# Delta rule in 32- and 48-row products on TensorE, with 16x16 inverses joined by products

## The reference

```python
k_n = k / (norm(k) + 1e-06)                  # batch 4, 8 heads, 768 tokens, head 48
for t in range(S):                           # the delta rule, state 48x48 per head
    y[t] = q[t] @ state
    v_old = state.T @ k_n[t]
    state = state + beta[t] * outer(k_n[t], v[t] - v_old)
x = y as (3072 tokens, 384)
h = x @ w_in;  x = (P(h) / (Q(h) + 1e-6)) @ w_out     # 384 -> 2048 -> 384, rational unit
h = x @ w_in2; out = (h * tanh(softplus(h))) @ w_out2 # same sizes
```

## Time and profile before

| | us |
|---|---|
| median of 3 runs | 1171.37 (1165.88 to 1178.27) |
| the profiled execution, its time | 1173.33 |
| its span | 1171.5 |
| TensorE, busy | 1071.8 (91%) |
| VectorE, busy | 950.9 (81%) |
| ScalarE, busy | 766.7 (65%) |
| GpSimd, busy | 171.6 (15%) |
| granted TensorE clock, mean | 0.943 of full speed |

### The profile page before, as it was taken

One profiled execution on the slowest core, in us unless ns is written; L12 is line 12 of the kernel. 1 busy time (PEld: TensorE's weight loads), 2 busy tenths in 40 slices (PEclk: granted clock), 3 DMA queues, 4 the chain that ended last, 5 costly groups with the idle time before them and its releaser, 6 DMA issues.

```text
span 1171.5 us, 22278 instructions
## 1 busy us (share of the span) xinstructions
PE 1071.8 (91%) x9321; PEld 870.6 (74%) x9366; DVE 950.9 (81%) x1045; ACT 766.7 (65%) x1039; POOL 171.6 (15%) x328
## 2 busy tenths in 40 slices
PE   5388999999888899999999999889999999999997
PEld 3276877877766677787787777668888888888885
DVE  4965567554569999999999999999887888878785
ACT  1535456466367687777867768687676767667664
POOL 2088787780000000000000000000000000000000
PEclk7588889996899999999999999999999999999999
DMA  7625447343021010000101003230010101010000
GB/s 198 185 62 159 137 111 192 97 110 124 22 87 54 1 55 1 25 30 0 54 0 54 1 1 108 81 107 28 1 55 1 54 0 54 1 54 1 25 4 27
DMA packets 30489, 69.03 MB, mean 59 GB/s; under 512 B 4160, under 2 KB 11840, under 8 KB 30400
## 3 DMA queue, kind: packets, MB, share of 16 engines
q1 hardware_dynamic: 30144, 66.98, 19.2%
q10 hardware_dynamic: 256, 0.79, 0.3%
HBM read 53.60 MB, written 14.16 MB: 58 GB/s over the span
## 4 chain that ended last, share of the span: by engine, by line
DVE 35%; PE 33%; issue 3%; ACT 2%; DVEq 0%; ACTq 0%
PE o_ps L837 6%; PE o_ps L838 5%; PE o_ps L839 5%; PE h_ps L837 5%; PE h_ps L839 5%; PE h_ps L838 5%; DVE val L1022 5%; DVE val L1041 5%; DVE val L1054 5%; DVE g_lo L1060 5%; DVE den L1014 5%; DVE den L1049 5%; DVE pa L1020 4%; PE h_ps L881 0%; ACT den L901 0%
## 5 line engine op out<-in xcount | busy, mean ns | idle before, releaser
L910 ACT ACTIVATE g_hi<-val 128x1024 fp32r<-128x1024 f32 x96 | 102.0, 1062 | 99.7 <-DVE val L1054 93.6
L837 PE MATMUL o_ps<-g_hi,w_hi_late 128*128 128x512 f32 x288 | 116.8, 405 | 20.5 <-DVE g_lo L1060 20.4
L837 PE MATMUL o_ps<-g_hi,w_hi_early 128*128 128x512 f32 x288 | 114.8, 399 | 14.3 <-ACT stage L947 9.2
L1054 DVE SCALAR_TENSOR_TENSOR val<-den,val 128x1024 f32<-128x1024 f32 x96 | 117.7, 1226 | 10.7 <-DVE den L1049 0.5
L1060 DVE SCALAR_TENSOR_TENSOR g_lo<-val,g_hi 128x1024 fp32r<-128x1024 f32 x96 | 117.6, 1225 | 1.6 <-ACT g_hi L910 1.5
L837 PE MATMUL h_ps<-x_hi,w_hi_early 128*128 128x512 f32 x288 | 112.2, 390 | 2.0 <-DVE val L1022 2.0
L837 PE MATMUL h_ps<-x_hi,w_hi_late 128*128 128x512 f32 x288 | 112.5, 391 | 1.6 <-DVE w_lo_late L88 1.6
L838 PE MATMUL o_ps<-g_lo,w_hi_late 128*128 128x512 f32 x288 | 113.8, 395 | 0.0
L839 PE MATMUL o_ps<-g_hi,w_lo_early 128*128 128x512 f32 x288 | 113.5, 394 | 0.0
L838 PE MATMUL o_ps<-g_lo,w_hi_early 128*128 128x512 f32 x288 | 113.4, 394 | 0.0
L839 PE MATMUL o_ps<-g_hi,w_lo_late 128*128 128x512 f32 x288 | 113.3, 393 | 0.0
(11 more groups left out here) (111 smaller groups left out, 2360.2 us busy)
## 6 DMA issues: line engine op xcount, KB each, us to landing
w_raw<-w SPq DMA_DIRECT2D x16, 768.0 KB, 6.1
kv_run<-kv_n SPq DMA_DIRECT2D x24, 384.0 KB, 4.6
x_raw<-x_dram SPq DMA_DIRECT2D x12, 768.0 KB, 5.8
kq_run<-kq_t SPq DMA_DIRECT2D x44, 192.0 KB, 3.5
kq_gram<-kq_t SPq DMA_DIRECT2D x40, 192.0 KB, 6.7
x_dram<-stage SPq DMA_DIRECT2D x24, 192.0 KB, 4.0
x_dram<-stage SPq DMA_DIRECT2D x6, 768.0 KB, 4.3
out<-stage SPq DMA_DIRECT2D x5, 768.0 KB, 4.1
```

The source lines that it names most:

```text
L837: nc.tensor.matmul(dst, hi, rhs_hi, start=first, stop=False)
L910: act_fn(g_hi[:, n % 2], val[:, n % 2], ACT.Copy, scale=-1.0).then_inc(g_hi_ready, 1)
L1054: dve_stt(val[:, e], den[:, e], 2.0, val[:, e], ALU.subtract, ALU.mult).then_inc(g_ready, 1)
```

## The change

The block-diagonal operands are gone. `solve`, `within` and the two halves of `update` work on the 32 rows of one batch at a time, 16 products each for 4 heads x 4 batches; `q_state` takes q as the loaded operand, so y comes out by token, in the upper half of the same two banks (`ky_ps`) that `k_state` writes. `turn_y` turns the y of the step before by two products with an identity matrix; ScalarE copies y before and after it. `update` is cut in halves with `turn_y` between them. Only the two diagonal 16x16 blocks are inverted by `substitute` (30 operations); the block between them is made by two rounds of products on TensorE (`join`, k = 0 and 1 for one half of the heads, 2 and 3 for the other) with a masked copy on ScalarE and a sum on VectorE. One buffer `kq` with three slots replaces `kq_gram` and `kq_run`, so k and q are loaded once. The warm products of the steps and the second burst are gone. `scale_gram` of tau 1 moves ahead of the first step. y is stored with one DMA for each half tau in place of two. In the diff, runs of removed lines are left out (the functions that held them are printed above), as are the first eight columns of indentation.

```diff
--- before.py
+++ after.py
...
+HC = C // 2
+BLK = HC * C + HC
 BANK = 512
+Y_AT = BANK // 2
...
-WARM = 2
...
+STEPS = 2 * (HC - 1)
+HALF = CG // 2
+def substitute(eng, tt, own, step, done):
+    n, x = blocks(n_turned), blocks(inv)
+    for r in range(HC - 1, 0, -1):
+        shape = [P, 2, r, HC - r]
+        prod = inv_t[:, own, :, 0:r, r:HC]
         if done:
             eng.wait_ge(step, done)
...
+        tt(prod, n[:, :, r, 0:r].unsqueeze(3).broadcast_to(shape),
+           x[:, :, r, r:HC].unsqueeze(2).broadcast_to(shape), ALU.mult).then_inc(step, 1)
         eng.wait_ge(step, done + 1)
-        tt(inv[:, j % 2, 0:r, r:C], inv[:, j % 2, 0:r, r:C], prod, ALU.subtract).then_inc(step, 1)
+        tt(x[:, :, 0:r, r:HC], x[:, :, 0:r, r:HC], prod, ALU.subtract).then_inc(step, 1)
...
+    load_kv(0, 0)
+    sp.wait_ge(ident_zeroed, 1)
+    for b in range(B):
+        sp.dma_start(ident[quad(b), quad(b)],
+                     consts[0:1, C + B:C + B + C * C].rearrange("o (i k) -> (o i) k", k=C)).then_inc(ident_loaded, 16)
+    load_norm(2)
...
+    def join(j, k):
+        h = k // 2
+        if k == 0:
+            pe.wait_ge(z_diag_ready, j + 1)
+            if j and j + 1 < T:
+                pe.wait_ge(gram_used, 4 * (j + 1) + 4)
+            elif j:
+                pe.wait_ge(joined, 2 * j)
+        elif k == 1:
+            pe.wait_ge(x_ready, TURNS * j + TURNS)
+            pe.wait_ge(r_ready, 2 * j + 1)
+        elif k == 2:
+            pe.wait_ge(joined, 2 * j + 1)
+        else:
+            pe.wait_ge(r_ready, 2 * j + 2)
+        by_event()
+        for n in range(HALF):
+            m = HALF * h + n
+            for b in range(B):
+                left, right = ((n_mat[quad(b), j % 2, m], z_diag[quad(b), m]) if k % 2 == 0 else
+                               (r_mat[quad(b), m], x_mat[quad(b), j % 2, m, HC:C]))
+                last = nc.tensor.matmul(side_ps[quad(b), HC * n:HC * n + HC], left, right, start=True, stop=True)
+        last.then_inc(join_done, 1)
...
         pe.wait_ge(state_ready, q + 1)
         by_event()
-        for u, r, v in slots:
+        for v in range(V):
             for b in range(B):
...
+                for r in range(HALVES):
+                    last = nc.tensor.matmul(ky_ps[quad(b), r, D * v:D * v + D],
+                                            kq[rows(r), slot(tau, c), 0, B * (V * g + v) + b],
+                                            state[rows(r), g, b % 2, b // 2, v],
+                                            start=(q == 0), stop=True, skip_group_check=True)
         last.then_inc(ks_done, 1)
...
     def solve(tau, c, g):
         q = index(tau, c, g)
...
+        if g == 0 and c % 2 == 0:
+            pe.wait_ge(joined, 2 * tau + c // 2 + 1)
+            by_event()
         pe.wait_ge(z_ready, q + 1)
         for u in range(U):
...
+            for b in range(B):
+                last = nc.tensor.matmul(hz_ps[quad(b), D * u:D * u + D],
+                                        x_mat[quad(b), tau % 2, HEADS * c + U * g + u],
+                                        z[quad(b), g, u], start=True, stop=True)
         last.then_inc(hz_done, 1)
+    def y_at(r, v, b):
+        return ky_ps[quad(b), r, Y_AT + D * v:Y_AT + D * v + D]
     def q_state(tau, c, g):
         q = index(tau, c, g)
-        pe.wait_ge(y_copied, q)
+        if q:
+            pe.wait_ge(y_copied, q)
+            by_event()
+        for v in range(V):
+            for b in range(B):
+                for r in range(HALVES):
+                    last = nc.tensor.matmul(y_at(r, v, b), kq[rows(r), slot(tau, c), 1, B * (V * g + v) + b],
+                                            state[rows(r), g, b % 2, b // 2, v],
+                                            start=(v == 0), stop=False, skip_group_check=True)
+        last.then_inc(q_done, 1)
+    def update(tau, c, g, h):
+        q = index(tau, c, g)
+        if h == 0:
+            pe.wait_ge(u_ready, q + 1)
+            pe.wait_ge(state_ready, q + 2)
+        else:
+            pe.wait_ge(st_half, q + 1)
         by_event()
-        for s in range(V * B):
+        for v in range(V):
             for r in range(HALVES):
...
+                for b in (2 * h, 2 * h + 1):
+                    at = V * D * h + D * v
+                    last = nc.tensor.matmul(st_ps[rows(r), b % 2, at:at + D],
+                                            kv_run[quad(b), c, 0, U * g + V * r + v],
+                                            u_row[quad(b), g, V * r + v], start=True, stop=True)
+        last.then_inc(st_done if h else st_half, 1)
     def within(tau, c, g):
         q = index(tau, c, g)
...
+        pe.wait_ge(q_done, q + 1)
+        if q + 1 < NQ * T:
+            pe.wait_ge(z_ready, q + 2)
+        by_event()
+        for v in range(V):
+            for r in range(HALVES):
+                for b in range(B):
+                    last = nc.tensor.matmul(y_at(r, v, b), p_mat[quad(b), tau % RING, HEADS * c + U * g + V * r + v],
+                                            u_row[quad(b), g, V * r + v],
+                                            start=False, stop=True, skip_group_check=True)
         last.then_inc(y_done, 1)
+    def turn_y(q):
+        pe.wait_ge(y_copied, q + 1)
+        if q == 0:
+            pe.wait_ge(ident_loaded, 16 * B)
+        else:
+            pe.wait_ge(t_copied, q)
+        by_event()
+        for r in range(HALVES):
+            last = nc.tensor.matmul(turn_ps[0:V * D, P * r:P * r + P], y_tok[:, q % 2, r], ident[:],
+                                    start=True, stop=True)
+        last.then_inc(t_done, 1)
...
+    keep_warm(side_ps[:], BURST)
+    join(0, 0)
+    join(0, 1)
+    pe.wait_ge(gram_used, 8)
     by_event()
     for tau in range(T):
         for s in range(NQ):
             c, g = s // G2, s % G2
...
+            q = index(tau, c, g)
             solve(tau, c, g)
...
+            if s < 2:
+                join(tau, 2 + s)
+            elif s < 6 and tau + 2 < T:
+                gram_fill(tau + 2, s - 2)
+            elif s >= 6 and tau + 1 < T:
+                join(tau + 1, s - 6)
             q_state(tau, c, g)
             if s + 1 < NQ:
                 k_state(tau, (s + 1) // G2, (s + 1) % G2)
             elif tau + 1 < T:
                 k_state(tau + 1, 0, 0)
...
+            update(tau, c, g, 0)
+            if q:
+                turn_y(q - 1)
+            update(tau, c, g, 1)
             within(tau, c, g)
+    turn_y(NQ * T - 1)
...
+    def masked(j, h):
+        act.wait_ge(join_done, joins_done(j, 2 * h))
+        nc.scalar.activation(r_mat[:, HALF * h:HALF * h + HALF, 0:HC],
+                             side_ps[:, 0:HALF * HC].rearrange("p (n k) -> p n k", k=HC),
+                             ACT.Copy, scale=lower_rows[:, 0:1]).then_inc(r_ready, 1)
     def copy_y(tau, c, g):
+        q = index(tau, c, g)
+        act.wait_ge(y_done, q + 1)
+        nc.scalar.activation(y_tok[:, q % 2], ky_ps[:, :, Y_AT:Y_AT + V * D], ACT.Copy).then_inc(y_copied, 1)
+    def copy_turned(q):
+        tau, c, g = q // NQ, q % NQ // G2, q % G2
         if c % 2 == 0 and g == 0:
...
+            act.wait_ge(hand.y_stored[c // 2], 16 * tau + 16)
+        act.wait_ge(t_done, q + 1)
+        nc.scalar.activation(y_stage[0:V * D, :, g, P * c:P * c + P],
+                             turn_ps[0:V * D, 0:HALVES * P].rearrange("p (r n) -> p r n", r=HALVES),
+                             ACT.Copy).then_inc(t_copied, 1)
...
+            if s == 0:
+                masked(tau, 1)
+            if s == 6 and tau + 1 < T:
+                masked(tau + 1, 0)
+            if (tau, s) == (0, 1):
                 roots(2)
...
+            if q:
+                copy_turned(q - 1)
+            copy_y(tau, c, g)
+            if c + 1 < CT:
+                scale_v(tau, c + 1, g)
             elif tau + 1 < T:
...
+                scale_v(tau + 1, 0, g)
...
+    def turn_z(j):
         if j:
             dve.wait_ge(inv_ready, j)
...
+            dve.wait_ge(join_done, joins_done(j - 1, 2))
+        nc.vector.transpose(z_diag[:].rearrange("p n i -> p i n"), square(inv)[:, 0:HC]).then_inc(z_diag_ready, 1)
+    def turn_x(j, a, b):
+        if j >= 2:
+            dve.wait_ge(hz_done, NQ * (j - 1))
+        nc.vector.transpose(x_mat[:, j % 2].rearrange("p n i -> p i n")[:, a:b],
+                            square(inv).rearrange("p k i -> p i k")[:, a:b]).then_inc(x_ready, 1)
+    def join(j, h):
+        dve.wait_ge(join_done, joins_done(j, 2 * h + 1))
+        dve.wait_ge(x_ready, TURNS * j + TURNS)
+        own = x_mat[:, j % 2, HALF * h:HALF * h + HALF, HC:C]
+        dve_tt(own, own, side_ps[:, 0:HALF * HC].rearrange("p (n k) -> p n k", k=HC), ALU.add).then_inc(joined, 1)
...
+        dve_tt(u_row[:, g], hz_ps[:, 0:U * D].rearrange("p (u d) -> p u d", u=U),
                wgt[:, tau, cg:cg + U].unsqueeze(2).broadcast_to([P, U, D]), ALU.mult).then_inc(u_ready, 1)
...
```

(89 more changed lines are left out.)

399 lines of the change are left out of this document (126 added, 273 removed).

## The result

The changed kernel takes 1311.41 us (median of 4 runs, 1308.07 to 1312.26) against 1174.82 for the kernel before on the same chip (4 runs): ratio 1.1186, 95% interval 1.1108 to 1.1263. One of the four runs before, 1189.01, fell in the slower of two states that executions of a kernel show here, and is left out of the ratio. It is 12% slower; the forecast was 1189 and its range ended at 1230.

A forecast was written before the change was run, and what follows sets the result against it. TensorE's own issue was taken as the bound, at half clock: 1173.3 + 24.5 (steps) - 8.2 (earlier start) + 1.1 (turn_y and copy behind) = 1190.7; that execution being 2 us above the median, 1189 us, range 1145 to 1230.

The forecast's parts named there:

- The sum of 288 us: The 48 steps of the stage, priced at 1.2 GHz: 288 us against 263.5 before, +24.5.
- third rival: In the stage TensorE runs short of instructions as records rise from 5,900 to 12,500; ends far above; chance 0.15.
- 15.6 ns a record: Half-clock price from k_state, 32 records in 0.50 us; also taken for q_state.
- The clock: In the steps: 1.2 GHz (granted 0.50) from shortly after the opening burst to the stage's end.
- The first rival: Clock stays at 2.4 GHz in the steps: 184 us for all, 1086 us in all; chance 0.08.
- C: Theory of the follow-up experiments: the loss is the half clock that small tiles and missing warm products bring.
- A plain step: Step without gram fill or join, summed group by group at half clock: 4.35 us.
- the two handovers: Around the copy of y between within and q_state: 0.15 us for both, in a 0.48 wait that solve hides.
- The second rival: Small tiles overlap better: update halves 0.25 us (20 us less), joins 1.3 (17 less), 1153 in all; chance 0.17.
- The change of tile shape: Idle time between groups of different tiles in a step: 0.33 us once, into turn_y, and four of 0.1.
- The start: Work ahead of the steps: first solve at 48.2 us, 8.2 earlier.
- steps 7: Last step of a tau: TensorE's join waits 0.8 us for x_mat, turned by VectorE; the step takes 7.15.

The follow-up runs named there:

- e1_unrolled: Kernel before with 1024 one-column products written out between the stage and the feed-forward: 1205.74 us; that group lasts 31.9 us.
- d1_no_loads: Changed kernel without the loads of k, q and v for later groups of tokens, old values being used again: 1297.92 us (one run).
- c1_warm8: Changed kernel with eight warm products put into each step, ahead of the first half of update: 1349.66 us.
- e2_loop: Kernel before with 1024 one-column products ahead of the feed-forward as a hardware loop, 32 rounds of 32: 1199.57 us; that group takes 16.0 us.
- b2_small_solve: Kernel before with only solve in 32x32 products, its spread operations on ScalarE gone: 1167.5 us, ratio 0.9929.
- a3_wide_join: Changed kernel with join products streaming 32 columns instead of 16, but for the last of each quad: 1305.69 us.

## Why the prediction was wrong

**The step that failed** is the supply of instructions. The sum of 288 us for the 48 steps has no term for it, on the ground that gram fills ran without a hole; it was left to the third rival, with a chance of 0.15, and the range ended 41 us above the forecast. That is room for 0.8 us for each of some 50 packets, and no run shows such a price: with 53 more packets over the span, 50 of them in the steps, there are 104.7 us of holes, 2.1 us for each of the 50, and that is nearly the whole miss: the steps took 120.1 us more than the 288, 107.6 of it idle time and 12.5 more work. The forecast's 15.6 ns a record is 2.0 us for 128 pairs, and its 288 us are 3.1 us for each of the 91.5 packets of the steps, while e1_unrolled, with hardly any work, got one in 3.46 to 3.74 us. A forecast by that pace alone would have had 91.5 x 3.5 = 320 us, too little again: measured are 408, 4.5 us a packet. That lies between the work of a packet (3.3 us busy) and this work plus a packet's 2.5 us (5.8), so part of each packet was hidden.

**What was held against it** didn't bear it: "gram fills at the full rate in the middle of the stage without such a hole". A fill of 64 pairs is half a packet, and the steps before need one only every 6.3 us, which leaves room for the 2.5 us of a packet. The row that spoke, 4.75 us with nothing to wait for the earlier trace rows, stood at the start, and I put it down to the loads. The DMA engines were full until 21 us, but TensorE went on only at 23.18, 2.6 us after the start of a packet of instructions at 20.54 (DMA share of the kernel before: 1.13 from 20 to 21 us, 0.48 and 0.05 in the two microseconds after). Without the later loads d1_no_loads gained 13 us only.

**The clock** was forecast rightly: 0.50 from the first steps to the end, but for 373 to 377 us. The 1.2 and 2.4 GHz of the texts ahead of the result answer to a pace that the warm products show: in c1_warm8 most of those that follow each other start 427 ns apart at a granted 0.50, 1.2 of their 512 columns a ns, and 216 ns apart at 1.0, 2.37 a ns. That the clock would stay low was my estimate from rows 4 (granted 1.00 from 184 to 189 us), 6 and 7 alone; no run shows which property of the products brings it down. The first rival (it stays) is refuted by the window; its step lengths add up to some 180 us and not 184, which changes nothing. C can't be the miss either, for the forecast had the half clock in it; the clock bought with eight warm products came out 38 us worse than none.

**The sum of the work** was near: 300.5 us busy against 288. A plain step at half clock is 4.49 to 4.69 (4.35). In it each group is followed by the next after: an update half 0.50 (0.46), turn_y 1.10 (0.70, 0.33 and 0.1), within 0.65 (0.50), solve 0.79 (0.50 and 0.1), q_state 0.33 to 0.37 and k_state 0.58 to 0.62 (0.50 each and one change). Joins are 50.7/24 = 2.1 us (2.0), the 1024 gram pairs in the steps 33.7/16 = 2.1 a fill (1.86). No row gives the forecast's 0.15 for the two handovers around the copy of y; at the end of the stage of the changed kernel they take 0.07 (within's end at 457.59 to the copy at 457.66) and 0.14 (its end at 457.99 to turn_y at 458.14). The second rival (better overlap) is refuted by the halves, 0.50 where it had 0.25, and by the joins, 2.1 where it had 1.3.

**The change of tile shape** is paid for, but not with 0.33 each. Solve's 32 records are followed after 0.79 by q_state, in 48-row tiles, and after 0.64 by a join in tiles of solve's own shape (382.98 and 383.62): 0.15 for the change. The starts of single records show it at all five changes of a step (from 422.2 to 427 us): 0.2 to 0.35 us from the last record of one group to the first of the next, against 0.04 to 0.06 between groups of one shape. The forecast allowed 0.33 once and 0.1 four times.

**The start** came at 49.97 (48.2, 56.44 before); 0.80 of the rest is a wait for z. GpSimd is busy for 61.8 us instead of 171.6, and no row of PE names it, as forecast. VectorE ended 1.1 us of PE's waits in the steps at x_mat, where I had 0.8 in each of the five steps 7; that the holes had given it time is likely and not shown.

**What stays open.** What starts a packet is not settled: in e1_unrolled it is the end of a burst, in the stage it comes anywhere from 2.2 us before TensorE's wait to 1.9 us into it, and the late ones are the long holes, up to 4.2 us. Nor is it shown what makes the clock fall.

## What to carry to other kernels

Before large products are cut into small ones, count pairs: in unrolled code every 128 pairs of load and product took a packet here (16.4 KB, 256 instructions), and TensorE could use one some 2.5 us after it had started to move (2.2 to 3.0 in the changed kernel). With 5.8 us of work a packet (the kernel before) next to nothing of that showed, with 3.3 (the changed kernel) 1.15 us did, with 1.14 (e1_unrolled) 2.3 to 2.6. A cut that saves work on the array but doubles the pairs can give the saving back there. A hardware loop took the borders away for one-column products (e2_loop); whether it does so for the real products, with their semaphores and changing addresses, no run here shows. The other way is to keep the small products where slow ones stand between: of the parts of this change only solve was tried alone, and it gains 0.7%, the best median of all that ran (b2_small_solve, 1167.5 us). Holes called "issue" that cut a group in its middle, 128 pairs after the last one, are the sign to look for.

## What the runs showed of the hardware

- With idle queues and unrolled one-column pairs, a packet of 256 instructions starts to move only as TensorE ends the one before, moves for 1.1 us, and is in use 2.3 to 2.6 us after its start: one packet in 3.46 to 3.74 us (e1_unrolled). In the changed kernel 69 holes end 2.2 to 3.0 us after a packet's start.
- The body of a loop, 32 pairs, was not brought again in 32 turns, and a turn cost some 0.16 us beside its products (e2_loop).
- One-column pairs in four 32-row tiles run at 8.9 ns each (128 in 1.14 us, e1_unrolled), when they are there.
- Joins of 32 columns took as long as joins of 16: 50.5 and 50.7 us for the 24 (a3_wide_join).
- In the changed kernel's steps, 408 us long, TensorE was granted 0.50 but for 373 to 377 us; with two warm products in a step, as in the kernel before (mean 0.86 in its steps), the changed kernel had 0.50 to 0.63 (a1_warm), and with eight 0.77 to 0.85 (c1_warm8). Without its two the kernel before had mostly 0.53 to 0.64 (b3_before_no_warm).
- 32 tiny products a step, 0.28 us of work, cost the kernel before 65 us: 13 are their own, 11 are holes, and the rest is longer work at a mean clock of 0.75 instead of 0.90 (49.9 to 458 us, b1_tiny_before).
